# The first four attention pairs of a fused attention and feed-forward kernel: the mask as a matrix product, another order on four engines, and one load on ScalarE's queue

## What is computed

```python
q_d, k_d, v_d = (t.reshape(B, H, S // 4, 4, D).mean(axis=3) for t in (q, k, v))
out_up = np.repeat(softmax_attention(q_d, k_d, v_d), 4, axis=2)
mask = np.abs(pos[:, None] - pos[None, :]) < 4
scores = np.where(mask, scale * q @ k.T, -1e9)
attn = exp(scores - max(scores)); attn = attn / (sum(attn) + 1e-9)
x = out_up + attn @ v                      # then [B*S, H*D]
h = x @ w_in1;  x = maximum(0.01 * h, h) @ w_out1
h = x @ w_in2;  out = (h - tanh(h)) @ w_out2
```

## Time and profile before

| | us |
|---|---|
| median of 3 runs | 960.08 (958.05 to 961.69) |
| the profiled execution, whole | 959.57 |
| its span, first to last instruction | 957.8 |
| PE busy in the span | 941.6 (98%) |
| DVE busy | 547.1 (57%) |
| ACT busy | 559.7 (58%) |
| POOL busy | 403.3 (42%) |

### The profile page before, as it was taken

How to read it: one execution, slowest core, us unless ns; L and a number is a source line. 1 busy time by engine, 2 the same in 40 slices (tenths; PEclk the granted TensorE clock), 3 DMA queues, 4 the chain that set the end, 5 groups by cost and what they waited for, 6 DMA issues and landing times.

```text
span 957.8 us, 19892 instructions
## 1 busy us (share of the span) xinstructions
PE 941.6 (98%) x7000; PEld 884.0 (92%) x7000; DVE 547.1 (57%) x1098; ACT 559.7 (58%) x1355; POOL 403.3 (42%) x343
## 2 busy tenths in 40 slices
PE   7999999999999999999999999999999999999998
PEld 6799999999999999999999998899899898898997
DVE  6755455535634544553235576776676766766764
ACT  4765546456446455364456677676666666656754
POOL 3584616327236246162442756433233332333232
PEclk9999999999999999999999999999999999999999
DMA  7875111211220121102003113000000000000000
GB/s 156 189 199 140 27 37 41 51 26 25 50 50 24 26 50 26 32 22 67 1 1 102 43 56 88 11 25 1 34 0 0 33 0 0 33 0 0 34 1 33
DMA packets 87797, 41.48 MB, mean 43 GB/s; under 512 B 60352, under 2 KB 81344, under 8 KB 87744
## 3 DMA queue, kind: packets, MB, share of 16 engines
q1 hardware_dynamic: 87744, 40.78, 16.2%
HBM read 36.04 MB, written 4.72 MB: 43 GB/s over the span
## 4 chain that ended last, share of the span: by engine, by line
PE 86%; POOL 4%; ACT 3%; issue 3%; DVE 2%; DMA 0%; SPq 0%; POOLq 0%; ACTq 0%; DVEq 0%
PE ph L531 13%; PE ph L532 13%; PE ph L533 13%; PE acc L607 7%; PE acc L608 7%; PE acc L609 7%; PE acc L560 6%; PE acc L561 6%; PE acc L562 6%; PE banks L429 2%; PE banks L461 2%; PE banks L448 2%; POOL in_lo L1127 1%; PE banks L422 1%; POOL pl L1111 1%
## 5 line engine op out<-in xcount | busy, mean ns | idle before, releaser
L1148 POOL TENSOR_TENSOR g_lo<-scratch,g_hi 128x384 fp32r<-128x384 f32 x96 | 125.8, 1311 | 257.8 <-ACT g_hi L734 257.8
L994 DVE TENSOR_TENSOR ph<-g,ph 128x288 f32<-128x288 f32 x128 | 58.9, 461 | 162.4 <-ACT g L748 161.8
L531 PE MATMUL ph<-x_hi,w_hi_a 128*128 128x288 f32 (+1 forms) x448 | 143.4, 320 | 0.8 <-DVE xT L884 0.5
L533 PE MATMUL ph<-x_hi,w_lo_a 128*128 128x288 f32 (+1 forms) x448 | 140.0, 312 | 0.0
L532 PE MATMUL ph<-x_lo,w_hi_a 128*128 128x288 f32 (+1 forms) x448 | 139.9, 312 | 0.0
L1127 POOL TENSOR_TENSOR in_lo<-w_whole,in_hi 128x512 fp32r<-128x512 f32 x64 | 82.5, 1289 | 131.0 <-ACT in_hi L714 131.0
L748 ACT ACTIVATE g<-ph 128x288 f32<-128x288 f32 x128 | 52.5, 410 | 130.9 <-PE ph L533 130.9
L1132 POOL TENSOR_TENSOR out_lo<-w_whole,out_hi 128x512 fp32r<-128x512 f32 x64 | 86.2, 1347 | 73.8 <-ACT out_hi L718 73.7
L1028 DVE SCALAR_TENSOR_TENSOR scratch<-scratch,ph 128x384 f32<-128x384 f32 x96 | 53.2, 554 | 110.7 <-ACT scratch L797 106.2
L796 ACT ACTIVATE scratch<-ph 128x384 f32<-128x384 f32 x96 | 46.8, 487 | 108.5 <-PE ph L533 106.9
L981 DVE TENSOR_TENSOR g_lo<-ph,g_hi 128x288 fp32r<-128x288 f32 x128 | 58.6, 458 | 59.1 <-ACT g_hi L734 59.1
(11 more groups left out here) (275 smaller groups left out, 2670.6 us busy)
## 6 DMA issues: line engine op xcount, KB each, us to landing
out_dram<-o_stage SPq DMA_DIRECT2D x18, 256.0 KB, 2.1
w_whole<-in_moe_w_in_dram SPq DMA_DIRECT2D x16, 256.0 KB, 3.8
w_whole<-in_moe_w_out_dram SPq DMA_DIRECT2D x16, 256.0 KB, 4.6
qn<-in_q_dram SPq DMA_DIRECT2D x26, 144.0 KB
kn<-in_k_dram SPq DMA_DIRECT2D x26, 144.0 KB
v4n<-in_v_dram SPq DMA_DIRECT2D x26, 144.0 KB
vw<-in_v_dram SPq DMA_DIRECT2D x26, 122.5 KB
scratch<-in_moe_w_in_dram SPq DMA_DIRECT2D x8, 256.0 KB, 2.8
```

Of the source, the lines that this page charges most:

```text
L531: pe.matmul(bank, whi, x_hi[:, c, 0:width], start=(c == 0), stop=False)
L533: last = pe.matmul(bank, wlo, x_hi[:, c, 0:width], start=False, stop=(c == CD - 1))
L1148: pool.tensor_tensor(g2_lo[:, f % 3, :], g2[:, f % 2, :], g2_hi[:, f % 3, :].bitcast(F32), ALU.subtract).then_inc(g_lo_done, 1)
```

## The change

- Mask: for the first four pairs PE multiplies the identity by `band` in float32r into each score bank (`put_mask`) and adds the scores to it (start=False). DVE no longer adds the mask; it takes the maximum of bank 0 straight from PSUM, sums k, and then subtracts and frees bank 0 in step 5, then bank 1. The hidden score becomes -2^26.
- Loads: A's k is issued by ACT's queue, ahead of its band copies; SP then goes from A's q to B's q. The kept weights 0 and 1 are issued between v's loads.
- Order: each engine gets its own exceptions to the order of `batch0`. DVE instead of ACT copies C's and D4's steps 12 and 14. The splits of x come later (slots 27 and 28), those of the kept weights have slots of their own for ACT and POOL. POOL's wait for A's subtraction goes, and D4's sum of v moves behind its step 10.
- Layer 1: the two hidden banks are swapped (`1 - f % 2`), so that the first hidden product goes into D4's bank 1 and starts before D4's bank 0 is free; the fills behind C's and D4's step 14 go, and C's step 3 gets two.

```diff
-KEPT_SLOTS = (24, 27)
-FILL = {("a", 1): 2, ("a", 3): 2, ("b", 1): 1, ("b", 3): 2, ("c", 14): 3, ("d", 14): 2}
-X_HI_SLOTS = {23: (0, 1), 27: (2,)}
-X_LO_SLOTS = {24: (0, 1), 27: (2,)}
+KEPT_HI_SLOTS = (22, 26)
+KEPT_LO_SLOTS = (24, 27)
+FILL = {("a", 1): 2, ("a", 3): 2, ("b", 1): 1, ("b", 3): 2, ("c", 3): 2}
+X_HI_SLOTS = {27: (0, 1), 28: (2,)}
+X_LO_SLOTS = {27: (0, 1), 28: (2,)}
...
+        def batch0(behind):
+            def placed(slot, at, s):
+                yield slot, at, s, 0
+                for (moved, step), place in behind.items():
+                    if place == (s, at):
+                        yield from placed(slot, step, moved)
...
+                    if (s, at) not in behind:
+                        yield from placed(slot, at, s)
...
-            load_qk(A, 0, 0)
+            load_q(A, 0, 0)
             load_qk(B, 0, 2)
...
             load_vw(B, 0, 2)
+            load_kept(0)
             load_vw(C, 0, 4)
+            load_kept(1)
             load_vw(D4, 0, 6)
-            load_kept(0)
-            load_kept(1)
...
+                                 start=not masked, stop=not masked or at == (NBA, NB - NBA)[bank] - 1)
...
+            def put_mask(s, bank):
+                n0, n1 = (0, NBA) if bank == 0 else (NBA, NB)
+                pe.matmul(s.banks[:, bank, 0:(n1 - n0) * WIN], ident_r[:, :], band_r[:, n0:n1, :],
+                          start=True, stop=False)
...
                 elif step == 4:
+                    pe.wait_ge(s.bank_free[1], uses1(i, 2))
+                    if first_of(i):
+                        pe.wait_ge(band_copied, 2)
+                        put_mask(s, 1)
                     pe.wait_ge(s.bank_free[0], uses0(i, 2))
-                    pe.wait_ge(s.bank_free[1], uses1(i, 2))
-                    scores(s)
+                    if first_of(i):
+                        put_mask(s, 0)
+                    scores(s, first_of(i))
...
-                hidden(ph1[:, f % 2, 0:T1], hi, lo, x1_hi, x1_lo, T1, CD * tile if f == 0 else None)
+                hidden(ph1[:, 1 - f % 2, 0:T1], hi, lo, x1_hi, x1_lo, T1, CD * tile if f == 0 else None)
...
-            for _, step, s, i in batch0():
+            for _, step, s, i in batch0({(A, 11): (C, 4), (B, 11): (D4, 4), (C, 15): (D4, 12), (C, 16): (D4, 14)}):
                 attention(step, s, i)
-                if s is C and step == 14:
-                    pe.wait_ge(A.bank_free[1], uses1(1, 0))
...
             for step in range(HEAD):
                 attention(step, A, 1)
-            for s in (B, C, D4):
+            pe.wait_ge(D4.bank_free[1], uses1(1, 0))
+            hidden1(0, 0)
+            pe.wait_ge(D4.bank_free[0], uses0(1, 0))
+            for s in (B, C):
                 pe.wait_ge(s.bank_free[0], uses0(1, 0))
                 pe.wait_ge(s.bank_free[1], uses1(1, 0))
-            layer1(0, CF, begun=False)
+            layer1(0, CF)
...
-                    if first_of(i):
-                        act.wait_ge(s.sub_l, 1)
-                    else:
-                        act.wait_ge(s.bank_free[1], uses1(i, 3))
+                    act.wait_ge(s.bank_free[1], uses1(i, 3))
                     act.activation(s.pl[:, :, :], s.pl[:, :, :], ACT.Exp, scale=L_SCALE).then_inc(s.exp_l, 1)
...
-                elif step == 12:
+                elif step == 12 and s not in (C, D4):
...
-                elif step == 14:
+                elif step == 14 and s not in (C, D4):
...
+            for h in range(2):
+                act.dma_start(A.kn[:, :, h, :], kv[:, h, :, :]).then_inc(A.k_loaded, 16)
...
-            for slot, step, s, i in batch0():
+            for slot, step, s, i in batch0({(D4, 7): (B, 15), (C, 15): (D4, 11)}):
...
                     if first_of(i):
-                        dve.tensor_tensor(s.pl[:, 0:NBA, :], half, band[:, 0:NBA, :], ALU.add)\
-                            .then_inc(s.bank_free[0], 1)
+                        dve.tensor_reduce(s.mxl[:, 0:NBA], half, AX_X, ALU.max).then_inc(s.max_half, 1)
...
-                elif step == 5 and first_of(i):
-                    dve.wait_ge(s.bank_full[1], uses1(i, 3))
-                    dve.tensor_tensor(s.pl[:, NBA:NB, :], local_scores(s, 1), band[:, NBA:NB, :], ALU.add)\
-                        .then_inc(s.bank_free[1], 1)
-                    dve.wait_ge(s.bank_free[1], uses1(i, 3))
-                    dve.tensor_reduce(s.mxl[:, :], s.pl[:, :, :], AX_X, ALU.max).then_inc(s.max_l, 1)
-                    dve.wait_ge(s.max_l, 1)
-                    dve.tensor_tensor(s.pl[:, :, :], s.pl[:, :, :], maxima(s, 0, NB), ALU.subtract)\
-                        .then_inc(s.sub_l, 1)
                 elif step == 5:
...
+                    if not first_of(i):
+                        dve.tensor_tensor(half, half, band[:, NBA:NB, :], ALU.add).then_inc(s.masked_half, 1)
+                    dve.wait_ge(s.max_half, 2 * i + 1)
                     dve.tensor_tensor(s.pl[:, 0:NBA, :], local_scores(s, 0), maxima(s, 0, NBA), ALU.subtract)\
                         .then_inc(s.bank_free[0], 1)
...
+                elif step == 12 and s in (C, D4):
+                    dve.wait_ge(s.bank_full[0], uses0(i, 5))
+                    dve.tensor_copy(s.pT[:, 4:8, :].rearrange("p n q -> p (n q)"), s.banks[0:WIN, 0, 0:4 * P])\
+                        .then_inc(s.bank_free[0], 1)
+                elif step == 14 and s in (C, D4):
+                    dve.wait_ge(s.bank_full[0], uses0(i, 6))
+                    dve.tensor_copy(s.pdT[:, 1, :], s.banks[0:HALF, 0, 0:QT * QP]).then_inc(s.bank_free[0], 1)
...
-            for slot, step, s, i in batch0():
+            for slot, step, s, i in batch0({(C, 12): (D4, 9), (A, 15): (C, 14), (A, 16): (A, 15),
+                                            (B, 15): (D4, 12), (B, 16): (B, 15), (C, 15): (B, 16),
+                                            (C, 16): (D4, 14)}):
...
-                    if first_of(i) and s is A:
-                        pool.wait_ge(A.sub_l, 1)
...
-            for slot, step, s, i in batch0():
-                if slot != done and kept_at(slot) is not None:
-                    split_kept(kept_at(slot))
+            for slot, step, s, i in batch0({(D4, 6): (D4, 10)}):
+                if slot != done and kept_at(KEPT_LO_SLOTS, slot) is not None:
+                    split_kept(kept_at(KEPT_LO_SLOTS, slot))
```

More of the change, by code:

```diff
@@ L187, in two_scale_attention_and_feed_forward @@
             A = PairBuffers("a", lambda name, shape: sb(name, shape, at=first), banks)
-            band = sb("band", [P, NB, WIN], at=first)
-            ident = sb("ident", [P, P], at=first)
+            band_r = sb("band", [P, NB, WIN], F32R, at=first)
+            ident_r = sb("ident", [P, P], F32R, at=first)
+            band, ident = band_r[:, :, :].bitcast(F32), ident_r[:, :].bitcast(F32)
             with ExitStack() as second:
@@ L313, in _, with load_q @@
         def _(sp):
-            def load_qk(s, i, head):
+            def load_q(s, i, head):
                 wait_from(sp, s.bank_full[0], uses0(i - 1, 2))
@@ L430, in score, with scores @@
                                  s.qT[keys, n * QB:n * QB + queries], s.kT[keys, n * QB:n * QB + WIN],
-                                 start=True, stop=True)
-            def scores(s):
+                                 start=not masked, stop=not masked or at == (NBA, NB - NBA)[bank] - 1)
+            def scores(s, masked):
                 for n in range(NBA - 1):
-                    score(s, 0, n, P if n == 0 else QB)
-                    score(s, 1, n)
-                score(s, 0, NBA - 1)
+                    score(s, 0, n, masked, P if n == 0 and not masked else QB)
+                    score(s, 1, n, masked)
+                score(s, 0, NBA - 1, masked)
                 for n in range(NBA, NB):
-                    last = score(s, 0, n)
+                    last = score(s, 0, n, masked)
                     if n == NB - 1:
                         last.then_inc(s.bank_full[1], 1)
-                    score(s, 1, n - 1)
-                score(s, 1, NB - 1).then_inc(s.bank_full[0], 1)
+                    score(s, 1, n - 1, masked)
+                score(s, 1, NB - 1, masked).then_inc(s.bank_full[0], 1)
+            def put_mask(s, bank):
+                n0, n1 = (0, NBA) if bank == 0 else (NBA, NB)
+                pe.matmul(s.banks[:, bank, 0:(n1 - n0) * WIN], ident_r[:, :], band_r[:, n0:n1, :],
+                          start=True, stop=False)
             def turn_l(s, bank, n0, n1):
@@ L629, in _ @@
             fill(8, ph1[:, 1, :])
[L630 removed]
+            for _, step, s, i in batch0({(A, 11): (C, 4), (B, 11): (D4, 4), (C, 15): (D4, 12), (C, 16): (D4, 14)}):
                 attention(step, s, i)
[L632 to L634 removed]
+                fill(FILL.get(("abcd"[FIRST.index(s)], step), 0), ph1[:, 1, :])
             for step in range(HEAD):
                 attention(step, A, 1)
[L637 removed]
+            pe.wait_ge(D4.bank_free[1], uses1(1, 0))
+            hidden1(0, 0)
```

(13 more changed lines are left out.)

46 lines of the change are left out of this document (22 added, 24 removed).

## The result

The change made the kernel slower: 965.48 us (median of 10 runs, 961.87 to 969.58) against 960.89 (10 runs of the kernel before beside it, 957.78 to 963.7), a ratio of 1.0057 with a 95% interval of 1.004 to 1.0073. The prediction was 958.0, its range ended at 960.9. A second series of the same kernel gave 1.0064 [1.0046, 1.0082]. The profiled execution took 961.87 us, its span 960.1, against 959.57 and 957.8 before: 2.3 us more.

A forecast was written before the change was run, and what follows sets the result against it. No engine is full; a chain of waits through the pipeline's fill bounds the first 50.2 us. D4's last combination -1.35 and the stretch to the first hidden product -0.27 give -1.6: 959.6 to 958.0 us, range 954.6 to 960.9.

The forecast's parts named there:

- First loads: Start, A's q and k: k's 0.56 us wait goes, q lands 0.2 us later; net -0.36 (bounds -0.56 and +1).
- rival 3: First loads: the new queue brings k no sooner, or q too late for A's scores to gain; 958.8 us, chance 0.15.
- Mask as a product: First four pairs: PE's product costs 0.2 us, A's scores -0.16; DVE saves 0.8 us a pair, C's scores at 20.45.
- The clock in the middle: Around C's scores: clock falls and rises as before (back at 26.0), scores take 2.92 us and end at 23.4, -0.2.
- rival 1: From 18.5 us: clock stays up or returns sooner, C's scores take 1.70 us; 956.0 us, chance 0.27.
- The exps: ACT's exps behind copies: DVE waits 1.0 us for B's; D4's sum still at 37.45 instead of 38.38, -0.93.
- The tail: Up to layer 1: two engines' gain and splits' cost even (-0.6 to +0.8); D4's last combination at 46.5, -1.35; then -0.27.
- Rival 2: Just before layer 1: without fills the clock falls at 45 us for 6.8 us, +3.4; 961.4 us, chance 0.13.
- All three signs: Sums wrong if C's scores take 1.7 us, q is waited for beyond 6 us, or clock under 1.00 after 26.

The follow-up runs named there:

- kernel 6: The kernel before with only A's k moved to ACT's queue; ratio 1.001 [0.9996, 1.0024].
- kernel 12: kernel 9 with A's k put back on ACT's queue, as the change has it; 957.06 us, ratio 0.9952.
- kernel 16: The program of kernel 12 run again, side by side with kernel 15; 956.36 us, ratio 0.995.
- kernel 2: The changed kernel with only A's k back on SyncE's queue behind q; median 962.78 us, ratio 1.0031.
- Kernel 8: The changed kernel with DVE's sums of the exps of A, B and C moved behind the next pair's subtraction (step 5); ratio 1.0025.
- kernel 9: The changed kernel with A's k on SyncE, POOL's work earlier, DVE's subtractions before exp sums, ACT's exps before late copies; 958.66 us, ratio 0.9972.
- kernel 1: The changed kernel with POOL waiting for all low parts of x before its second kept split; median 965.08 us, ratio 1.0044.
- kernel 4: The changed kernel with eight fill products on PE before the first hidden product; median 966.51 us, ratio 1.0074.
- kernel 5: The changed kernel again, unaltered; ratio 1.0064 [1.0046, 1.0082].
- kernel 15: kernel 9 run again, with A's k on SyncE's queue; 958.69 us, ratio 0.9962.
- 10: The kernel before with the mask as a product and DVE's subtractions of B, C, D4 before the preceding pair's exp sums; ratio 1.0009.
- 13: kernel 9 with only ACT's order put back as the change has it; 960.75 us, ratio 0.999.
- 14: kernel 9 with only POOL's order put back as the change has it; 960.84 us, ratio 0.9988.

## Why the prediction was wrong

**First loads.** Forecast: q 0.2 us later, k's wait gone, -0.36. Measured: q 0.7 us later, k's turn 0.06 later. The term was mis-sized, inside its bounds (up to +1), and rival 3 was right for this stage. So was the rule of the Trainium skill that it cites ("DMA: Bandwidth & Descriptors", section "Issuing engines are not separate DMA queues"); the rows go further, since q comes later too. In the nine profiles with k on SyncE's queue q's turn starts at 5.12 to 5.71, in the nine with k on ACT's at 5.80 to 6.92. DMA engines that are 0.70 busy over a window say little of how full they are while q lands: from 3.5 to 4.5 us they were 0.60 busy before and 0.94 after. In the time it cost nothing that could be told in the kernel before (kernel 6) and was no loss in the mended one (12 and 16); in the change itself it may have cost some 0.3% (kernel 2).

**Mask as a product.** Forecast 0.2 us (bounds 0.1 and 0.5). From k's turn to the scores it takes 1.70 us instead of 1.37: 0.33. What I left out works the other way: the scores themselves take 1.38 us instead of 1.69, since the two products with a 64x128 weight load (the form 64*128, up to 325 ns long where the others take 221) are gone, so the first maximum starts at 10.65 against 10.57. DVE does save its 0.6 to 0.8 us. That it loses it again at bank 0 was forecast, but too small: A's step 6, which stands between B's turns of k on PE as before, now waits for DVE's subtraction of bank 0 and starts at 12.54 instead of 11.81, and B's scores start at 14.66 instead of 13.61 (+1.05, forecast +0.45); B's step 6 starts at 19.09 (18.45), C's scores at 22.25 (20.45), being also behind the two new fills and at the lower clock. Kernel 8 bounds what undoing that wait is worth.

**The clock in the middle.** Forecast to fall and rise as before; it fell at 19.5 as before but was back at 23.0 instead of 26.0. C's scores took 1.71 us, so half of rival 1 came true and made up for their late start: they end at 23.96, before at 23.61.

**The exps.** The mechanism is as forecast: DVE waits for B's and C's exp 0.50 us each and 1.22 for D4's, D4's sum starts at 38.05 (38.38 before, forecast 37.45). Only the size was off, by the 0.6 us of late scores.

**The tail is the step that failed.** "Gain of two engines and cost of the splits I put at even": D4's last combination ends at 50.58 instead of 46.5, and of these 4.1 us only 0.6 were brought along from D4's sum, so 3.5 are this step's, far outside its bounds (+0.8). Two things are in it.

The largest is the hold of 2.5 us (3.00 against 0.45): the splits of x lie on POOL's splits of the kept weight. I had the rule in hand and used it one step earlier, for a 0.56 us operation: the Trainium skill ("SBUF — State Buffer", section "Who interferes with whom") has VectorE and GpSimd share a port pair that one of them holds for a whole instruction. The row here goes further: the hold outlasts one instruction of POOL (2.36 us) and lasts until the second of two back to back is done. The trace of before gave the means to see it, in the row of x 3's split above: 1.01 us for an operation of 0.46, beside POOL's split of 46.67 to 49.03. The change moved the splits of x 0 and 1 from slot 24 to 27, onto POOL's second kept split, and the high part of kept 1 from 27 to 26, so that POOL goes straight on from the first to the second. Laying the two engines' new orders side by side was what the working lacked.

The second is the hold of 0.85 us ahead of C's step 12. The prediction took 0.39 us as gained because POOL no longer worked beside D4's step 8; that came true (0.17 us for the operation of 0.56), but POOL's next product then lay beside D4's step 9.

The two holds come to 3.4 of the 3.5 us, an estimate from one trace. In kernel 9 the held operations take 0.61 us (D4's step 9) and 1.22 us (the two splits of x) instead of 1.05 and 3.37.

What looks like a third loss is mostly the order itself. C's last combination comes at 45.50 instead of 43.23 although D4's sum starts 0.3 us earlier than before, since in DVE's new order C's step 12 stands behind D4's step 9: from the start of D4's sum to that combination it takes 7.45 us in the change and 7.44 in kernel 9, against 4.85 before. What follows is shorter in return, from there to the first g 4.67 us in kernel 1 and 4.84 in kernel 9, against 6.93 before. Kernel 9 has the combination at 42.50 because its earlier scores and exps bring D4's sum to 35.06.

**The clock in the tail.** Rival 2 had the place, and its cause fits the traces: the clock fell behind PE's wait of 1.95 us, and stayed up in the two profiles in which that wait is gone (kernel 1) or filled with products (kernel 4, whose fills stand in another place than those that the change took away). Its price does not fit. From the last three hidden products to the first g it takes 1.13 us in the change and 0.89 in kernels 1 and 4, so up to there the fall cost 0.24 us of the 3.4 that rival 2 allows. In kernel 5's profile, where the clock was low from 48.7 to 55.6, the second g came another 1.1 us late. That rival 2's 961.4 lies close to the profiled 961.87 is luck.

**The signs and the chances.** All three signs that the prediction named for wrong sums came: C's scores took 1.71 us, q was waited for beyond 6 us, and the clock was under 1.00 after 26. The chance of slower by over 0.5%, 0.03, was far too low. I counted each loss in one execution, and not that executions of one kernel differ in how long their clock is low in the first 60 us; in both series of the change the mean clock (0.9915, 0.9932) lies below that of every series of the kernel before (0.9941 to 0.9958). Whether the new idle time is what causes that was not shown.

## What to carry to other kernels

When operations are moved, lay the new order of VectorE and GpSimd side by side and look for SBUF-to-SBUF work of the one over long SBUF work of the other: here 4.69 us of the one held an operation of 0.45 us of the other for 3.00. Less work on an engine is worth nothing while its order keeps the next engine waiting; an order is a set, and parts that won nothing when put into the kernel before (mask, mask with DVE's order, k's queue) were in kernels that won 0.3 to 0.5%. And a short idle stretch of TensorE can be dearer than it looks, where the clock falls behind it: against kernel 16, the profile of kernel 15 has 1.4 us more of waiting and 3.5 us more at the first hidden product. Where the work behind the fall waits for another engine anyway, as in the change's tail, it cost 0.24 us.

## What the hardware showed beyond that

How fast q's turns run differs from execution to execution of one kernel: eight of them took 0.72 to 0.88 us in twelve profiles and 1.17 to 1.22 in those of 4, 8, 10, 12, 13 and 14 (kernels 12 and 16 are the same program, with 1.22 and 0.72), though the granted clock in the records is 1.00 there. Even so kernel 12, whose profile has such a start, ran at a mean clock of 0.9996 over its twelve executions, the highest of all that were measured.
